# Two readiness counts for a routed expert's weight slot, zero rows issued around the first routed tile, and gate products spread between layer products

## What is computed

```python
x = chunked_softmax_attention(q, k, v)         # 4 x 8 heads, 576 positions, chunks of 64
x = hardswish_layer(x, w_in, w_out)            # 2304 tokens, 512 -> 2048 -> 512
logits = x @ w_gate
noisy = logits + log1p(exp(x @ w_noise)) * noise
top2, weights = two_best(noisy), softmax_over_them   # of 8 experts
for e in range(8):                             # each token goes to two experts
    h = maximum(x[of e] @ w1[e], 0)            # 512 -> 1024
    out[of e] += weight * (h @ w2[e])          # 1024 -> 512
```

## Time and profile before

| | before |
|---|---|
| median of three executions | 1037.46 us (1037.05 to 1038.91) |
| the profiled execution | 1037.52 us |
| its span, first to last instruction | 1035.8 us |
| outside the span | 1.7 us |
| PE busy in the span | 965.1 us (93%) |
| POOL busy | 515.8 us (50%) |
| DVE, ACT busy | 521.0 us, 322.4 us |
| mean granted clock of PE | 0.97 |

### The profile page before, as it was taken

The page is one execution under the profiler, slowest core; times in us unless marked ns, Lnnn a source line. Parts: engine busy times, 40 slices in busy tenths (PEclk is TensorE's granted clock), DMA queues, the critical chain, the costliest instruction groups (busy, mean ns, idle before and its releaser), DMA issues.

```text
span 1035.8 us, 18247 instructions
## 1 busy us (share of the span) xinstructions
PE 965.1 (93%) x5864; PEld 852.3 (82%) x5865; DVE 521.0 (50%) x942; ACT 322.4 (31%) x446; POOL 515.8 (50%) x743
## 2 busy tenths in 40 slices
PE   6999999999999999999699979699696996999996
PEld 6999999999999999998488758588585885878884
DVE  5554455565565556636556435345244443544344
ACT  3223333332422432323133323233132332333222
POOL 6994002002002002987636848758488484972445
PEclk9999999999999999999899989899899998999999
DMA  8342324423332433845565746646456465447839
GB/s 339 137 157 72 82 92 122 114 72 133 103 102 103 103 107 111 261 153 122 192 164 132 167 107 163 152 123 158 123 134 160 119 169 137 101 91 154 187 106 314
DMA packets 193895, 145.99 MB, mean 141 GB/s; under 512 B 159920, under 2 KB 160048, under 8 KB 193840
## 3 DMA queue, kind: packets, MB, share of 16 engines
q1 hardware_dynamic: 175360, 89.94, 34.5%
q0 software_dynamic: 12288, 44.05, 13.5%
q10 hardware_dynamic: 6192, 11.27, 3.0%
HBM read 65.80 MB, written 40.63 MB: 103 GB/s over the span
## 4 chain that ended last, share of the span: by engine, by line
PE 60%; POOL 32%; issue 3%; DMA 2%; SPq 2%; POOLq 1%; DVE 0%; ACT 0%; DVEq 0%
PE ps L1319 17%; POOL W L546 13%; PE ps L1306 12%; PE ps L1333 11%; PE ps L1418 10%; POOL W L542 8%; PE ps L1337 6%; POOL W L499 5%; POOL W L496 3%; POOL y_hi L584 2%; PE ps L1347 1%; POOL EXraw L529 1%; POOLq L521 1%; PE ps L1275 1%; PE ps L1254 1%
## 5 line engine op out<-in xcount | busy, mean ns | idle before, releaser
L1306 PE MATMUL ps<-W,xg_part 128*128 (+1 forms) x1032 | 262.8, 412 | 49.6 <-POOLq L553 39.6
L1306 PEld LDWEIGHTS ps<-W,xg_part 128*128 128x128 f32 x1032 | 202.9, 198 | 101.6 <-issue 52.4
L1418 PE MATMUL ps<-W,hT_part 128*128 (+1 forms) x1032 | 247.2, 395 | 1.2 <-ACT hT_part L764 1.2
L1418 PEld LDWEIGHTS ps<-W,hT_part 128*128 128x128 f32 x1032 | 194.2, 188 | 47.0 <-issue 1.7
L1319 PE MATMUL ps<-x_part,W 128*128 128x384 f32 x1152 | 223.5, 343 | 3.3 <-POOL W L499 2.8
L1319 PEld LDWEIGHTS ps<-x_part,W 128*128 128x128 f32 x1152 | 202.1, 189 | 6.5 <-POOL W L499 4.6
L546 POOL TENSOR_TENSOR W<-EXraw,W 128x256 fp32r<-128x256 f32 x224 | 193.8, 895 | 4.7
L509 POOL DMA_INDIRECT routed_x<-x_halves,slot_blk x30 | 29.6, 988 | 294.6 <-DVE slot_blk L922 286.1
L542 POOL TENSOR_SCALAR W<-EXraw 128x256 fp32r<-128x256 f32 x224 | 108.6, 510 | 95.3 <-PE ps L1418 88.7
L1333 PE MATMUL ps<-g_part,W 128*128 128x384 f32 x768 | 149.7, 337 | 0.0
L1333 PEld LDWEIGHTS ps<-g_part,W 128*128 128x128 f32 x768 | 135.4, 188 | 0.3 <-ACT g_part L628 0.2
(11 more groups left out here) (180 smaller groups left out, 748.2 us busy)
## 6 DMA issues: line engine op xcount, KB each, us to landing
EXraw<-in_w POOLq DMA_DIRECT2D x24, 1024.0 KB, 6.3
QKV<-qkv SPq DMA_DIRECT2D x15, 768.0 KB, 4.8
routed_y<-y_sb ACTq DMA_DIRECT2D x43, 256.0 KB, 2.0
routed_y<-zero_tile SPq DMA_DIRECT2D x14, 768.0 KB, 4.0
Wraw<-w_moe SPq DMA_DIRECT2D x16, 512.0 KB, 8.2
EXraw<-in_w SPq DMA_DIRECT2D x8, 1024.0 KB, 5.6
out<-y_lo SPq DMA_DIRECT2D x18, 256.0 KB, 3.4
routed_x<-zero_tile SPq DMA_DIRECT2D x8, 256.0 KB, 2.1
```

The source lines that it names most:

```text
L1306: last = nc.tensor.matmul(dst, a(ha), b(hb), start=(i == 0), stop=(i == n - 1))
L1418: last = nc.tensor.matmul(ps[:, 4, :], hT_part[hh][:, n, :], W[hw][:, weights(slot, W1W + n * DM, DM)], start=(n == 0 and k == 0), stop=(n ...
```

## The change

Three things are changed.

1. The count `ex_ready` becomes `ex_up_ready` and `ex_down_ready`. From the third expert in order on POOL splits parts 0 to 3 once the *up* product of the last tile of expert p - 2 is done (`eh_ready`), and parts 4 to 7 once its *down* product is (`y_ready`). `expert_up` waits for the first count and `expert_down` for the second, for which it reads `need_tab` once more.
2. On SP all eight entries of `order_tab` are read ahead of the wait for `pads_ready`; three zero-row transfers stand ahead of `turn_x(3)` and five behind it.
3. The gate products of a block's tiles stand apart: behind `up(1)`, `down(0)` and `up(2)`; for the last block inside the four steps of `up_half(0, 1, 0)`. For the last block DVE and ACT take their steps in another order too (`merge_x(2)` behind gate part 3, `hidden_low(0)` between parts 1 and 2, `softplus` ahead of `hidden_high(0)`).

The core of the diff (the declarations of the counts are left out):

```diff
...
@@ -434,10 +434,12 @@
             turn_early(2)
             turn_rows(NB - 1)
 
+            experts = [sp.value_load(order_tab[0:1, p:p + 1], min_val=0, max_val=E - 1) for p in range(E)]
             sp.wait_ge(pads_ready, 1)
-            for p in range(E):
-                e = sp.value_load(order_tab[0:1, p:p + 1], min_val=0, max_val=E - 1)
-                row = sp.value_load(pad_row[0:1, bass.ds(e, 1)], min_val=0, max_val=(E - 1) * CAP + N)
+
+            def pad(p):
+
+                row = sp.value_load(pad_row[0:1, bass.ds(experts[p], 1)], min_val=0, max_val=(E - 1) * CAP + N)
                 sp.dma_start(xs[bass.ds(row, P), :], zero_tile[:].bitcast(U16)).then_inc(padded[p], 16)
 
             def turn_x(g):
@@ -456,6 +458,8 @@
                 sp.sem_inc(wait_carrier, 1)
                 sp.dma_start_transpose(out=hT_halves[s][:], in_=h_halves[s][:]).then_inc(halves_turned[s], 16)
 
+            for p in range(3):
+                pad(p)
             sp.wait_ge(tab_ready, 1)
             for n in range(2):
                 sp.wait_ge(scattered_late[n], SCATTERS)
@@ -464,6 +468,9 @@
                 for p in range((0, 2, 3)[g - EARLY], (2, 3, E)[g - EARLY]):
                     sp.wait_ge(padded[p], 16)
                 turn_x(g)
+                if g == EARLY:
+                    for p in range(3, E):
+                        pad(p)
             for s in range(2):
                 turn_half(EARLY, s, first=True)
             turn_x(2 * EARLY)
@@ -528,7 +535,7 @@
                     dst = raw.rearrange("p (n f) -> p n f", f=DM)
                 nc.gpsimd.dma_start(dst, src).then_inc(ex_fetched[c], 16)
 
-            def split_expert(p, parts=range(8)):
+            def split_expert(p, parts):
                 for c in parts:
                     at_w = (p % 2) * SLOT
                     if c % 2 == 0 and p == 1:
@@ -548,9 +555,8 @@
                     if c % 2 == 1 and p + 1 < E:
                         pool.wait_ge(ex_taken, SUB // NARROW * (8 * (p - 1) + c + 1))
                         load_expert(p + 1, c // 2)
-                if parts[-1] == 7:
-                    pool.wait_ge(ex_taken, SUB // NARROW * 8 * p)
-                    pool.sem_inc(ex_ready, 1)
+                pool.wait_ge(ex_taken, SUB // NARROW * (8 * (p - 1) + parts[-1] + 1))
+                pool.sem_inc(ex_up_ready if parts[-1] < 4 else ex_down_ready, 1)
 
             def split_first(c):
                 if c % 2 == 0:
@@ -566,19 +572,23 @@
             for c in range(8):
                 split_first(c)
             pool.wait_ge(first_taken, 8 * SUB // NARROW)
-            pool.sem_inc(ex_ready, 1)
+            pool.sem_inc(ex_up_ready, 1)
+            pool.sem_inc(ex_down_ready, 1)
             scatter(NB - 2, 0)
-            split_expert(1, range(AHEAD))
+            split_expert(1, range(4))
             scatter(NB - 1, 1)
             pool.wait_ge(places_ready, 1)
             pool.wait_ge(scattered_late[1], SCATTERS)
-            split_expert(1, range(AHEAD, 8))
+            split_expert(1, range(4, 8))
             for p in range(2, E):
 
                 done = pool.value_load(done_tab[0:1, p - 2:p - 1], min_val=1, max_val=G)
+                pool.wait_ge(eh_ready, done)
+                pool.sem_inc(wait_carrier, 1)
+                split_expert(p, range(4))
                 pool.wait_ge(y_ready, done)
                 pool.sem_inc(wait_carrier, 1)
-                split_expert(p)
+                split_expert(p, range(4, 8))
 
             def gather(t, s, dst, got):
                 nc.gpsimd.indirect_dma_start(
@@ -712,8 +722,8 @@
             take_x1T(NB)
             hidden(0)
             xg_high(1)
+            softplus(NB - 1)
             hidden_high(0)
-            softplus(NB - 1)
             hidden(1)
             xg_high(2)
             weight_ratio(NB - 1)
@@ -1158,13 +1168,14 @@
             take_x1T(NB)
             halve_x1(NB - 1, 0)
             halve_x1(NB - 1, 1)
+            halve_x1(NB - 1, 2)
+            gate(NB - 1, 0, ATT)
             xg_low(1)
+            gate(NB - 1, 1, ATT)
+            hidden_low(0)
+            gate(NB - 1, 2, ATT)
+            gate(NB - 1, 3, ATT)
             merge_x(2)
-            gate(NB - 1, 0, ATT)
-            halve_x1(NB - 1, 2)
-            hidden_low(0)
-            for part in range(1, 4):
-                gate(NB - 1, part, ATT)
             xg_low(2)
             rows_of_block(NB - 1, 1, ATT)
             dve.wait_ge(slots_step, 7 * NB)
@@ -1297,13 +1308,13 @@
                 mix_values(t, first_src[t], PROLOGUE_BANK[t])
             keep_busy(WARM_LONG)
 
-            def product(dst, terms):
+            def product(dst, terms, opens=True, closes=True):
 
                 last, n = None, len(terms) * len(PASSES)
                 i = 0
                 for a, b in terms:
                     for ha, hb in PASSES:
-                        last = nc.tensor.matmul(dst, a(ha), b(hb), start=(i == 0), stop=(i == n - 1))
+                        last = nc.tensor.matmul(dst, a(ha), b(hb), start=(opens and i == 0), stop=(closes and i == n - 1))
                         i += 1
                 return last
 
@@ -1369,10 +1380,10 @@
                     return 0
                 return pe.value_load(slot_tab[0:1, bass.ds(g, 1)], min_val=0, max_val=SLOT)
 
-            def up_half(g, s, slot):
+            def up_half(g, s, slot, range_of_k=range(KD)):
                 terms = [(lambda c, n=n: xg_part[c][:, n, :],
-                          lambda c, n=n: W[c][:, weights(slot, n * F2 + s * BANK, BANK)]) for n in range(KD)]
-                return product(ps[:, s, :], terms)
+                          lambda c, n=n: W[c][:, weights(slot, n * F2 + s * BANK, BANK)]) for n in range_of_k]
+                return product(ps[:, s, :], terms, range_of_k[0] == 0, range_of_k[-1] == KD - 1)
 
             def h_residual(g):
                 pe.wait_ge(hh_ready, g + 1)
@@ -1385,7 +1396,7 @@
                 slot = expert_slot(g)
                 if not isinstance(g, int) or g >= EARLY:
                     need = pe.value_load(need_tab[0:1, bass.ds(g, 1)], min_val=1, max_val=E)
-                    pe.wait_ge(ex_ready, need)
+                    pe.wait_ge(ex_up_ready, need)
                 pe.wait_ge(xgh_ready, g + 1)
                 pe.wait_ge(xgl_ready, g + 1)
                 for s in range(F2 // BANK):
@@ -1407,6 +1418,9 @@
 
             def expert_down(g, between=None):
                 slot = expert_slot(g)
+                if not isinstance(g, int) or g >= EARLY:
+                    need = pe.value_load(need_tab[0:1, bass.ds(g, 1)], min_val=1, max_val=E)
+                    pe.wait_ge(ex_down_ready, need)
                 pe.wait_ge(hh_ready, g + 1)
                 pe.wait_ge(hl_ready, g + 1)
                 if not isinstance(g, int) or g > 0:
@@ -1423,16 +1437,19 @@
                 first = not gate
                 for f in range(NF):
                     up(i, f, par, first)
+                    if gate and f == 1:
+                        if i > 1:
+                            pe.wait_ge(slots_ready, i - 1)
+                        x1_logits(i - 1, 0, ATT)
+                    if gate and f == 2:
+                        x1_logits(i - 1, 2, ATT)
                     if f > 0:
                         down(i, f - 1, first)
                     elif not first:
                         down(i - 1, NF - 1, False)
                     if gate:
                         if f == 1:
-                            if i > 1:
-                                pe.wait_ge(slots_ready, i - 1)
-                            for t in range(TB):
-                                x1_logits(i - 1, t, ATT)
+                            x1_logits(i - 1, 1, ATT)
                         if f == RANKS_AT[not attend]:
                             if attend:
                                 pe.wait_ge(xl_ready, TB * i + 2 * TB)
@@ -1458,9 +1475,12 @@
             up_half(0, 0, 0)
             down(NB - 1, NF - 1, False)
             pe.wait_ge(g_done, NF * NB)
-            up_half(0, 1, 0).then_inc(eh_ready, 1)
-            for t in range(TB):
-                x1_logits(NB - 1, t, ATT)
+            up_half(0, 1, 0, range(0, 2))
+            x1_logits(NB - 1, 0, ATT)
+            x1_logits(NB - 1, 1, ATT)
+            up_half(0, 1, 0, range(2, 3))
+            x1_logits(NB - 1, 2, ATT)
+            up_half(0, 1, 0, range(3, 4)).then_inc(eh_ready, 1)
             hidden_transpose(0)
             expert_up(1)
             pe.wait_ge(first_taken, 8 * SUB // NARROW)
```

4 lines of the change are left out of this document (2 added, 2 removed).

## The result

The changed kernel takes 996.51 us (median of four executions, 989.21 to 997.23); the kernel before took 1038.18 us on the same chip (1037.05 to 1040.54). The ratio is 0.958, with a 95% interval from 0.9532 to 0.9628. So it is faster, as forecast, but by 41.7 us and not by 57.9: the forecast was 979.6, its range ended at 987.0. The profiled execution took 996.31 us with a span of 994.7; before it was 1037.52 and 1035.8, so the two traces differ by 41.1 us.

What follows compares the result with a forecast made beforehand. PE was taken as idle for POOL's weight split: a loop of 65.9 us where five tiles need 55.9. Gains of 51.1 + 6.0 + 0.8 = 57.9 from 1037.5 gave 979.6 us, range 973.5 to 987.

Steps and rivals of the forecast that it cites:

- Part 1, the stalls: Routed loop: with two counts all six stretches over a change of expert take 11.18 us each, 51.1 us less.
- U: End of expert p-2's last up product; new up product at U + 50.3, down at U + 67.1, slack 24 and 15 us.
- the five stretches: Down product ahead of a change of expert to the next down product: 21.59 to 20.81 us, 106.69 us together.
- Part 2: Zero rows ahead of the routed loop: first turn 7.0 us earlier; 2.4 us cover tile 3's later half turns.
- rival 5: Slower: VectorE's chain sets the tile pitch as POOL never pauses; 1050 us at 2.2 us a tile, chance 0.02.
- line 1213 ending after the down product could start: Sign of a wrong forecast: DVE's line 1213 ends after the down product could start.
- The table reads: PE's added need_tab read and wait ahead of each down product, hidden by queued matmuls: 0 us.
- VectorE beside POOL: VectorE's steps slowed wherever POOL now works, not enough to show on PE: 0 us.
- Zero rows and first tile: First routed tile, with the last block's gate order: turn starts at 503.6, 6.0 us less, between 3.6 and 9.4.
- the blocks' clock: Second block behind gate products: spreading them may keep PE's clock up, 0.8 us less, between 0 and 1.7.
- the first up product's restart: Routed loop's first up product: restart cost falls from 2.45 to 1.6 us, 0.9 less.
- The end: Last gathers behind the stores of tiles 34 and 39 keep their distance to PE's tiles: no change.

Runs made afterwards that it cites:

- first_loads: Changed kernel with expert 2's last two loads moved later, the third quarter's behind tile 3's landed half turn: 992.72 us, ratio 0.9547.
- loads_later: Changed kernel with the first three quarters' loads, from expert 2's split on, issued behind the next part's high pieces: 989.33 us, ratio 0.9545.
- all_loads: Changed kernel with the load moves of first_loads and loads_later together: 982.39 us, ratio 0.9446.
- all_loads_gates: all_loads with gate products and the last block's steps in the order of the kernel before: 980.86 us, ratio 0.945.
- counts_only: Kernel before with only the two counts and their two waits, zero rows and gate products as before: 997.94 us, ratio 0.9645.
- gates_before: Changed kernel with gate products and the last block's steps in the order of before: 992.28 us, ratio 0.9562.
- pads8: Changed kernel with all eight zero-row transfers ahead of the first routed turn (tile 3's): 993.02 us, ratio 0.9575.

## Why the prediction was wrong

Point by point, by its own steps:

1. **Part 1, the stalls (51.1 us).** The mechanism was right: no wait of the up product for POOL, 11.18 us a tile through the changes of expert, POOL waiting for PE in between (32.1 us). The slack was stated one tile off: the first up product of the new expert starts at U + 61.5 and not U + 50.3, and its down product at U + 78.2, so there are 35 and 26 us of slack. It did no harm. Two readings were off without consequence: the five stretches last 20.81 to 22.21 us, not up to 21.59, and 52.0, 8.1 and 5.6 are 65.7.
2. **The step that failed** is the sum's silence on the transfers: "All six stretches should then take 11.18 us each" took each half turn at 3.2 us and asked only what POOL and PE wait for. The cover of 2.4 us in Part 2 was about right (3.24 + 2.4 = 5.6; the waits of this trace have covers of 5.8 to 6.2), but it was weighed against SP's order at tile 3 alone and against VectorE's steps in rival 5, not against the weight loads, which move with POOL's split. The trace of before had turns of 6.0 to 6.5 us in the last tile ahead of each of the five stalls, hidden behind the wait of the earlier trace rows that was to go. The missing term is 15.3 us in the profiled execution (51.1 - 35.8). The rivals had the right victim (line 1213 ending after the down product could start) and the wrong cause.
3. **The table reads (0)** were right: PE makes them all and keeps 11.18 us a tile wherever nothing else is late.
4. **VectorE beside POOL (0)** was right for the sum, though not for each step. DVE is busy for 520.5 us (521.0 before) and the low part takes 1.29 us on average (1.30 before), with POOL now working through. But single steps did grow beside POOL's pieces: the low part to 2.33 us once in the changed kernel and to 4.18 us in first_loads, where it made a wait of 1.65 us; the copy of `xT_halves`, 0.8 us, to 4.8 us once each in loads_later, all_loads and all_loads_gates, where the merge behind it waited for the turn anyway. By the exclusive lock of the Trainium skill (SBUF — State Buffer, Who interferes with whom) a step of VectorE with two SBUF inputs, as the low part has, can be held up for a whole instruction of GpSimd that reads SBUF. The 4.18 us agree in kind, though 3 us more are several of POOL's instructions (0.5 and 0.9 us each), and the means show that most steps weren't held up.
5. **Zero rows and first tile (6.0) with the blocks' clock (0.8).** 6.8 forecast and 6.8 measured, but from other parts. The turn started at 501.37 (503.6 forecast): the gate chain was quicker than worked out (`chosen` done at 486.36 instead of 488.4, first step on the ranks at 488.34 instead of 490.55). 1.4 us of it stem from the blocks' clock, in the forecast 0.8. And the first up product's restart stayed at 8.13 us (8.05 before), where 0.9 us less were forecast.
6. **The end (0)** took 1.6 us more. POOL's last gathers, which set the end of the chain, take 0.95 us mostly; two of them took 4.45 and 5.03 us here, where before one took 6.36. VectorE was busy nearly throughout at that time in both traces, but what stretched them wasn't tried.

Why it still came out on the right side: the stalls removed were 51 us, and a new wait is only what a slow turn exceeds its cover by: at the worst turn of all, 11.1 us, that was 4.9 us, and an expert issues four loads.

The Trainium skill has a sentence on the failed step, which was not weighed in the prediction: by DMA: Bandwidth & Descriptors (Issuing engines are not separate DMA queues), DMAs of the scalar, sync or gpsimd engine "will ultimately run on the same 16 DMA engines and interleave with each other, regardless of the engine that started them". The rows of 654 to 662 agree, with both queues at 39.0% and 35.3%. If a turn and a load shared the engines' time evenly, a turn of 3.2 us would grow to 6.4 at most; most of the rows of the table stay near that, the six between +0.05 and +0.25 with a median of 9.32 do not. The 159 packets of 256 bytes against 132 of 4 KB, from 659 to 661.5, would fit a sharing packet by packet, in which the queue with the small packets loses most. That is an argument from one window and not shown: from 661.5 to 663.5 it was 501 against 70.

**Left open.** Why a load that is issued just behind the copy's end is worse than one issued with it; when POOL's pieces hold up a step of VectorE for 3 us or more; and the last waits of all_loads, in the splits of experts 2 and 3, with loads issued 3.2 us (0.4 us of wait), 0.03 us (0.8) and 0.2 us (1.9) ahead of a copy's end, which weren't moved further.

## What to carry to other kernels

A long wait is also a cover. Before a wait is taken away, look for what was already late behind it: here turns of 6.0 to 6.5 us stood in the trace of before, harmless for 8 us of stall. When an edit moves an engine's work, list the transfers that it issues and lay their new times against the short transfers that others wait for; here two loads issued 4 to 6 us later and the rest moved by a few tenths gave back some 11 us. And a kernel whose executions spread over 1.3% where its neighbours spread over 0.3% to 0.5% may have such a near miss in it; compare two of its own profiles.

## What the runs showed of the hardware that was not expected

A turn of 256 KB (128 x 1024 elements of two bytes) from SP took 3.2 us alone and up to 11.1 us with one 1 MB load from POOL beside it, and the effect has a sharp edge: at 0.25 to 0.45 us the median is 6.36, at 0.45 to 1.2 us it is 3.28, though three of those fifteen turns still took over 6 us.

A step of VectorE of 0.8 to 1.2 us took 4.2 to 4.8 us beside POOL's pieces in four of twelve traces, with the same instructions on both engines throughout.

The clock behind gate products depends on how they stand. The stretch from 106 to 110 us, by windows (stretch, busy times, granted clock, DMA), in counts_only, all_loads_gates and the changed kernel:

```profile
106.00:110.00 4.00, 4.00 (x16) 4.00 (x16) 0.00 (x0) 0.23 (x1) 0.00 (x0) 0.58 0.00 0
```

```profile
106.00:110.00 4.00, 4.00 (x17) 4.00 (x16) 0.08 (x1) 0.58 (x1) 0.00 (x0) 0.63 0.00 0
```

```profile
106.00:110.00 4.00, 4.00 (x28) 4.00 (x27) 1.26 (x3) 1.10 (x2) 0.00 (x0) 1.00 0.00 0
```

With the products together it was at 0.57, 0.58 and 0.63 in three of four profiles and at 1.00 in gates_before; with the products spread it was at 1.00 in all eight. So spreading them seems to be what keeps it up, with one grouped run against it, and it is worth some 1.4 us. The rule of the Trainium skill that the prediction named (TensorE: Matmul & The Clock Gate, Part 1) agrees: by it spreading could only help. At 478.5 to 485.5, behind the last block's gate, the clock was 0.78 before and 0.82, 0.81 and 0.76 in all_loads_gates, loads_later and pads8 and 1.00 in the other eight, so spread products do not always keep it there.
